# Second feed-forward on one core: VectorE takes the third pair's first sums between two softmaxes, and GpSimd waits for a tile's norm ahead of the next low part

## The chip, the cores and the metric

One core of a Trainium2 chip runs the whole program. The metric is the device time of one execution in microseconds (us), the median of the runs; less is better. A difference of under 0.2% (1.8 us here) counts as no change.

## The reference, cut to what matters

Attention with a decaying state gives 3072 tokens of 512 numbers. The first feed-forward follows (512 to 2048, ELU, back to 512), and then the second one, which the change is about:

```python
h = x @ w_in                                   # 3072 x 512 @ 512 x 1024
e = np.exp(h - np.max(h, axis=-1, keepdims=True))
solu = h * e / (np.sum(e, axis=-1, keepdims=True) + 1e-09)
mu = np.mean(solu, axis=-1, keepdims=True)
var = np.mean((solu - mu) ** 2, axis=-1, keepdims=True)
ln = (solu - mu) / np.sqrt(var + 1e-06) * g_ln
return ln @ w_out                              # 1024 x 512
```

## The kernel before, in words

Every matmul of the feed-forwards is split: an operand is a high part (rounded to the matmul's format by a ScalarE copy) plus a low part (the rest, a subtraction on VectorE or GpSimd), and each product is three matmuls: high with high, high with low, low with high.

The second feed-forward goes over 12 pairs of tiles of 128 tokens, `u` or `p` for a pair and `t` for a tile. Its first matmul is done by a scheme with seven products in place of eight for the four quarters of `h` (Strassen's, in Winograd's form). Products and sums of a pair `u` are these:

- TensorE, `up_product` (L513 to L521), six matmuls each: `opening_products` (P1 into bank X, P6 into bank Y), `middle_products` (P2 into X, P5 into W, then P7 into Y, which waits for the sum U2), `last_products` (P4 into Y, which waits for the sum U3, then P3 into W, which waits for H22).
- ScalarE copies P1 out (`copy_p1`, L925) and the first quarter of `h` (`copy_h2`, L932).
- VectorE, `add` (L710 to L712): `first_sums` makes U2 from P1 and bank Y, U3 from P1 and Y after P7, and H22 from U3 and bank W. `last_sums` makes H21 and H12.

Then each tile goes through `solu_max` (L816, L818), the exponential on ScalarE (L980), `solu_product` (L823), `solu_moments` (L829 to L838), the reciprocal root on GpSimd (`rstd`, L393) and `solu_normalise` (L845, L847, L849). TensorE transposes it (`norm_transposes`, L593, banks 4 and 5), ScalarE copies the high part (L990), VectorE takes the low part (`normalised_lo`, L805), and `solu_down` (L607 to L609, two halves of 12 matmuls) multiplies by the second weights.

Each engine runs its own list in the order written. TensorE's for a pair `p`, which makes the products of pair `p+1` between the transposes of tiles `2p` and `2p+1`, is: opening products, middle products, transposes of `2p`, last products, transposes of `2p+1`, four halves of `solu_down`. At `p = 0` the first tile's `solu_down` comes ahead of the transposes of tile 1, and the opening products of pair 2 follow those; at `p = 1` the list so begins with the middle products of pair 2. `norm_transposes(t)` waits for the tile's norm (semaphore `soft`, 13 counts for each tile) and for both low parts of the tile before (`nl_done`), since they are read from the same banks. VectorE's list has all of `first_sums(p+1)` at the start of pair `p`, behind both softmaxes of the pair before.

GpSimd makes the four sums of the input of a pair (`sum_x2`, L375, L378, L380, L383) and its low part (`split_x2_lo`, L388), both from SBUF, between the `rstd` of tiles. The low part also frees `x2_raw`, on which SyncE's load of the next input waits (`load_x2`, L299). Its sums come next in GpSimd's list, ahead of the next pair's two `rstd`.

Of the kernel before, what the change touches and what calls it, by code (L numbers as in the profile page):

```python
# [21 lines left out]
NT = TOK // P  # L22
NPAIR = NT // 2
# [10 lines left out]
def build(nc, units, w1, w_in2, w_out2, g_ln, tables, x2_dram, out):  # L34
# [4 lines left out]
    with ctx:  # L39
# [190 lines left out]
        SOFT = 13  # L230
# [9 lines left out]
        def sums(u, i):  # L240
            return 5 * u + i
# [105 lines left out]
        @block.gpsimd  # L347
        def _(pool):
            nc.gpsimd.memset(warm[:, :], 0.0).then_inc(warm_zeroed, 1)
            nc.gpsimd.memset(minus_half[:, :], -0.5).then_inc(consts_set, 1)  # L350

            def decay_q(n):
                pool.wait_ge(qk_in[slot(n)], 16 * loads(n))
                qt = tile_of(n)[:, QT]
                nc.gpsimd.tensor_tensor(qt, qt, q_decay[:, :], ALU.mult).then_inc(q_decayed, 1)  # L355

            def decay_v(n):
                pool.wait_ge(kv_in[slot(n)], 16 * loads(n))
                v = tile_of(n)[:, VN].rearrange("p (h d) -> p h d", d=D)
                nc.gpsimd.tensor_tensor(v, v, v_decay[:, :].unsqueeze(2).to_broadcast([P, H, D]), ALU.mult)\  # L360
                    .then_inc(v_decayed, 1)

            pool.wait_ge(q_decay_in, 16)
            decay_q(0)
            pool.wait_ge(v_decay_in, 16)
            decay_v(0)
            for n in range(1, NCH):
                decay_q(n)
                decay_v(n)

            def sum_x2(u):

                z = 4 * u
                pool.wait_ge(x2_in, 16 * (u + 1))
                nc.gpsimd.tensor_tensor(x2_raw[:, S3, :], x2_raw[:, A11, :], x2_raw[:, S1, :], ALU.subtract)\  # L375
                    .then_inc(x2_summed, 1)
                pool.wait_ge(x2_summed, z + 1)
                nc.gpsimd.tensor_tensor(x2_raw[:, S1, :], x2_raw[:, S1, :], x2_raw[:, A22, :], ALU.add).then_inc(x2_summed, 1)  # L378
                pool.wait_ge(x2_summed, z + 2)
                nc.gpsimd.tensor_tensor(x2_raw[:, S2, :], x2_raw[:, S1, :], x2_raw[:, A11, :], ALU.subtract)\  # L380
                    .then_inc(x2_summed, 1)
                pool.wait_ge(x2_summed, z + 3)
                nc.gpsimd.tensor_tensor(x2_raw[:, S4, :], x2_raw[:, A12, :], x2_raw[:, S2, :], ALU.subtract)\  # L383
                    .then_inc(x2_summed, 1)

            def split_x2_lo(u):
                pool.wait_ge(x2h_done, u + 1)
                nc.gpsimd.tensor_tensor(x2_lo[u % 2], x2_raw, x2_hi[u % 2].bitcast(f32), ALU.subtract).then_inc(x2l_done, 1)  # L388

            def rstd(t):  # L390
                par = t % 2
                pool.wait_ge(soft[par], SOFT * (t // 2) + 10)
                nc.gpsimd.tensor_tensor(stats[par][:, 8:9], stats[par][:, 7:8], minus_half[:, :], ALU.pow)\  # L393
                    .then_inc(rstd_done[par], 1)

            def scale_w4(k):
                pool.wait_ge(w4_in[k], 16)
                part = w_raw[:, W4 + 2 * k:W4 + 2 * k + 2, :]
                nc.gpsimd.tensor_tensor(part, part, gln_sb[:, 2 * k:2 * k + 2].unsqueeze(2).to_broadcast([P, 2, 512]),
                                        ALU.mult).then_inc(w4_scaled, 1)  # L400

            pool.wait_ge(consts_set, 1)
            pool.wait_ge(gln_in, 32)
            sum_x2(0)
            split_x2_lo(0)
            sum_x2(1)
            split_x2_lo(1)
            for k in range(4):
                scale_w4(k)
            sum_x2(2)  # L410
            split_x2_lo(2)
            rstd(0)
            rstd(1)
            for p in range(NPAIR - 1):
                if 0 < p < NPAIR - 2:
                    split_x2_lo(p + 2)
                if p + 3 < NPAIR:
                    sum_x2(p + 3)
                rstd(2 * p + 2)
                rstd(2 * p + 3)  # L420
# [225 lines left out]
        def _(dve):  # L646
# [63 lines left out]
            def add(out_, u, i, kept, bank, needs):  # L710
                dve.wait_ge(product, products(u, needs))
                nc.vector.tensor_tensor(out_, kept, bank, ALU.add).then_inc(h2_summed, 1)  # L712
# [83 lines left out]
            def last_sums(u):  # L796

                add(h2[:, 1, 0:512], u, H21, p1[:, :], Y, P4)
                add(h2[:, 0, 512:1024], u, H12, u2[:, :], W, P3)

            def normalised_lo(t):
                for q in range(2):
                    dve.wait_ge(nh_done, 2 * t + q + 1)
                    part = slice(q * (NF2 // 2), (q + 1) * (NF2 // 2))
                    nc.vector.tensor_tensor(n_lo[:, t % 2, part, :], ps[:, 4 + q, :].rearrange("p (f t) -> p f t", t=P),  # L805
                                            n_hi[:, t % 2, part, :].bitcast(f32), ALU.subtract).then_inc(nl_done, 1)
# [4 lines left out]
            def solu_max(t):  # L811
                u, done = t // 2, soft[t % 2]
                if t % 2 == 0:
                    dve.wait_ge(h2_copied, u + 1)
                dve.wait_ge(h2_summed, sums(u, H12))
                nc.vector.reduce_max(column(t, 0), h2[:, t % 2, :], AX.X).then_inc(done, 1)  # L816
                dve.wait_ge(done, SOFT * u + 1)
                nc.vector.tensor_scalar(column(t, 1), column(t, 0), -1.0, None, ALU.mult).then_inc(done, 1)  # L818

            def solu_product(t):  # L820
                par = t % 2
                dve.wait_ge(exp_done[par], t // 2 + 1)
                nc.vector.tensor_tensor(e3[:, par, :], e3[:, par, :], h2[:, par, :], ALU.mult).then_inc(soft[par], 1)  # L823

            def solu_moments(t):
                u, par, done = t // 2, t % 2, soft[t % 2]
                z = SOFT * u
                esum, esum_eps, r, r2, v = (column(t, n) for n in (2, 3, 4, 5, 7))
                nc.vector.tensor_scalar(esum_eps, esum, EPS_SM, None, ALU.add).then_inc(done, 1)  # L829
                dve.wait_ge(done, z + 4)  # L830
                nc.vector.reciprocal(r, esum_eps).then_inc(done, 1)
                for q in range(2):
                    nc.vector.bn_stats(bn[par][:, 6 * q:6 * q + 6], e3[:, par, 512 * q:512 * q + 512]).then_inc(done, 1)
                dve.wait_ge(done, z + 7)
                nc.vector.tensor_tensor(r2, r, r, ALU.mult).then_inc(done, 1)
                nc.vector.bn_aggr(mv[par][:, :], bn[par][:, :]).then_inc(done, 1)
                dve.wait_ge(done, z + 9)
                nc.vector.tensor_scalar(v, mv[par][:, 1:2], r2, EPS_LN, ALU.mult, ALU.add).then_inc(done, 1)  # L838

            def solu_normalise(t):  # L840
                u, par, done = t // 2, t % 2, soft[t % 2]
                z = SOFT * u
                r, rs, a, nb = (column(t, n) for n in (4, 8, 9, 10))
                dve.wait_ge(rstd_done[par], u + 1)
                nc.vector.tensor_tensor(a, rs, r, ALU.mult).then_inc(done, 1)  # L845
                dve.wait_ge(done, z + 11)
                nc.vector.tensor_scalar(nb, mv[par][:, 0:1], a, -1.0, ALU.mult, ALU.mult).then_inc(done, 1)  # L847
                dve.wait_ge(done, z + 12)
                nc.vector.tensor_scalar(e3[:, par, :], e3[:, par, :], a, nb, ALU.mult, ALU.add).then_inc(done, 1)  # L849
# [18 lines left out]
            add(h2[:, 1, 0:512], 1, H21, p1[:, :], Y, P4)  # L868
            solu_normalise(1)
            add(h2[:, 0, 512:1024], 1, H12, u2[:, :], W, P3)  # L870
            for p in range(NPAIR):
                t = 2 * p
                if 0 < p:
                    if p < NPAIR - 1:
                        first_sums(p + 1)
                        normalised_lo(t)
                        last_sums(p + 1)
                normalised_lo(t + 1)
                if p < NPAIR - 1:
                    solu_max(t + 2)  # L880
                    solu_max(t + 3)
                    for n in (t + 2, t + 3):
                        solu_product(n)
                        solu_moments(n)
                        if n == NT - 1:
                            normalised_lo(NT - 2)
                        solu_normalise(n)

        @block.scalar
        def _(act):  # L890
# [217 lines left out]
```

## Time and profile before

| what | value |
|---|---|
| median of 3 runs | 900.86 us (900.52 to 901.19) |
| the profiled execution | 900.97 us, of which the span is 899.2 us |
| TensorE matmul busy | 882.3 us (98%) |
| VectorE busy | 454.7 us (51%) |
| ScalarE busy | 327.7 us (36%) |
| GpSimd busy | 171.2 us (19%) |
| granted TensorE clock, mean over the span | 0.994 |

1.77 us of the profiled execution lie outside the span. Busy shares are means over the whole span; the change touches the stretch from about 630 us on.

### The profile page before, as it was taken

The numbers are of one execution on the slowest core, as the hardware profiler recorded it, in microseconds if no ns is written. First come the engines' busy times: TensorE is split into PE (matmuls) and PEld (weight loads), VectorE is DVE, ScalarE is ACT, GpSimd is POOL, SyncE is SP. The second block draws the span as 40 slices with busy tenths as digits, with TensorE's granted clock in tenths as the row PEclk, the third lists the DMA queues.
The fourth block names the chain that finished last, engine by engine and source line by source line (L and its number), as shares of the span: only waits on it lengthen the run. The fifth ranks groups of instructions, "written<-read, shape, count | busy, mean of one in ns | idle before, by whom it ended". The sixth has DMA issues, their size and how long they took to land.

```text
span 899.2 us, 12162 instructions
## 1 busy us (share of the span) xinstructions
PE 882.3 (98%) x4998; PEld 719.1 (80%) x4998; DVE 454.7 (51%) x755; ACT 327.7 (36%) x524; POOL 171.2 (19%) x142
## 2 busy tenths in 40 slices
PE   8999999999999999999999999999969999999998
PEld 5788888888888888888888888888858888888886
DVE  4765533332423332233423333485877777777774
ACT  2545332322423233332323244653323333333332
POOL 4221101110101111110200025211133333333200
PEclk9999999999999999999999999999979999999999
DMA  9900131110400131110400022401101111111001
GB/s 345 408 30 33 47 94 47 47 49 1 141 23 26 47 94 47 47 47 1 141 1 1 1 71 71 163 1 36 51 32 47 48 47 48 47 48 47 24 24 47
DMA packets 34006, 57.80 MB, mean 64 GB/s; under 512 B 2848, under 2 KB 15392, under 8 KB 33952
## 3 DMA queue, kind: packets, MB, share of 16 engines
q1 hardware_dynamic: 33376, 56.70, 18.2%
q8 instruction: 39, 0.64, 0.3%
q10 hardware_dynamic: 576, 0.33, 0.1%
q14 instruction: 15, 0.12, 0.0%
HBM read 44.44 MB, written 12.58 MB: 63 GB/s over the span
## 4 chain that ended last, share of the span: by engine, by line
PE 94%; DVE 4%; POOL 1%; issue 1%; DMA 0%; ACT 0%; POOLq 0%; ACTq 0%
PE ps L506 11%; PE ps L510 10%; PE ps L507 10%; PE ps L484 10%; PE ps L485 9%; PE ps L490 9%; PE ps L607 4%; PE ps L609 4%; PE ps L608 4%; PE ps L518 4%; PE ps L520 4%; PE ps L519 4%; PE ps L438 3%; PE ps L469 3%; PE ps L593 2%; PE ps L466 1%
## 5 line engine op out<-in xcount | busy, mean ns | idle before, releaser
L732 DVE TENSOR_TENSOR g_lo<-e,g_hi 128x512 fp32r<-128x512 f32 x96 | 76.7, 799 | 168.5 <-ACT g_hi L951 168.2
L506 PE MATMUL ps<-g_hi,w_hi 128*128 128x512 f32 x384 | 154.1, 401 | 0.0
L484 PE MATMUL ps<-x_hi,w_hi 128*128 128x512 f32 x384 | 149.9, 390 | 0.9 <-ACT x_hi L908 0.7
L510 PE MATMUL ps<-g_lo,w_hi 128*128 128x512 f32 x384 | 150.0, 391 | 0.0
L507 PE MATMUL ps<-g_hi,w_lo 128*128 128x512 f32 x384 | 149.7, 390 | 0.0
L485 PE MATMUL ps<-x_hi,w_lo 128*128 128x512 f32 x384 | 149.5, 389 | 0.0
L951 ACT ACTIVATE g_hi<-e 128x512 fp32r<-128x512 f32 x96 | 60.7, 632 | 202.7 <-PE ps L510 184.6
L725 DVE SCALAR_TENSOR_TENSOR e<-e,ps 128x512 f32<-128x512 f32 x96 | 65.7, 684 | 132.0 <-ACT e L942 132.0
L940 ACT ACTIVATE e<-ps 128x512 f32<-128x512 f32 x96 | 57.3, 597 | 141.9 <-PE ps L490 141.1
L355 POOL TENSOR_TENSOR tiles<-tiles,q_decay 128x512 f32<-128x512 f32 x23 | 31.8, 1383 | 384.1 <-DMA tiles<-units_dram 378.1
L490 PE MATMUL ps<-x_lo,w_hi 128*128 128x512 f32 x384 | 102.6, 389 | 0.0
L506 PEld LDWEIGHTS ps<-g_hi,w_hi 128*128 128x128 f32 x384 | 72.1, 188 | 17.9 <-issue 0.7
L484 PEld LDWEIGHTS ps<-x_hi,w_hi 128*128 128x128 f32 x384 | 72.1, 188 | 16.8 <-ACT x_hi L908 0.9
L510 PEld LDWEIGHTS ps<-g_lo,w_hi 128*128 128x128 f32 x384 | 72.1, 188 | 15.4
L490 PEld LDWEIGHTS ps<-x_lo,w_hi 128*128 128x128 f32 x384 | 72.1, 188 | 14.9
L485 PEld LDWEIGHTS ps<-x_hi,w_lo 128*128 128x128 f32 x384 | 72.1, 188 | 14.8
L507 PEld LDWEIGHTS ps<-g_hi,w_lo 128*128 128x128 f32 x384 | 72.2, 188 | 14.0
L607 PE MATMUL ps<-w_hi,n_hi 128*128 128x512 f32 x192 | 76.1, 396 | 0.0
L518 PE MATMUL ps<-w_hi,x_hi 128*128 128x512 f32 x168 | 67.7, 403 | 8.3 <-DVE u L712 8.3
L609 PE MATMUL ps<-w_hi,n_lo 128*128 128x512 f32 x192 | 75.0, 390 | 0.0
L608 PE MATMUL ps<-w_lo,n_hi 128*128 128x512 f32 x192 | 74.7, 389 | 0.0
L520 PE MATMUL ps<-w_hi,x_lo 128*128 128x512 f32 x168 | 66.1, 393 | 0.0
(84 smaller groups left out, 1165.2 us busy)
## 6 DMA issues: line engine op xcount, KB each, us to landing
tiles<-units_dram SPq DMA_DIRECT2D x46, 512.0 KB, 4.8
w_raw<-w_dram SPq DMA_DIRECT2D x32, 256.0 KB, 10.0
x_between<-x SPq DMA_DIRECT2D x24, 256.0 KB, 2.7
x_raw<-x_between SPq DMA_DIRECT2D x12, 512.0 KB, 3.5
out_dram<-y_sb SPq DMA_DIRECT2D x24, 256.0 KB, 2.0
w_raw<-w_out_dram SPq DMA_DIRECT2D x4, 512.0 KB, 3.7
w_raw<-w_in_dram SPq DMA_DIRECT2D x4, 512.0 KB, 5.3
tile<-units_dram SPq DMA_DIRECT2D x2, 512.0 KB, 10.9
```

Source lines behind the costliest of these rows:

```text
L484: nc.tensor.matmul(bank, hi, x_hi[:, j % 2, k, :], start=(k == 0), stop=False)
L485: nc.tensor.matmul(bank, lo, x_hi[:, j % 2, k, :], start=False, stop=False)
L490: last = nc.tensor.matmul(bank, hi, x_lo[:, j % 2, k, :], start=False, stop=(k == KD - 1))
L506: nc.tensor.matmul(ps[:, 4 + m, :], hi, g_hi[:, f % 2, :], start=(f == 0), stop=False)
L507: nc.tensor.matmul(ps[:, 4 + m, :], lo, g_hi[:, f % 2, :], start=False, stop=False)
L510: last = nc.tensor.matmul(ps[:, 4 + m, :], hi, g_lo[:, f % 2, :], start=False, stop=(f == NF1 - 1))
L518: nc.tensor.matmul(bank, x_h, hi, start=(first and k == 0), stop=False, skip_group_check=True)
L520: done = nc.tensor.matmul(bank, x_l, hi, start=False, stop=(k == 1), skip_group_check=True)
L607: nc.tensor.matmul(bank, n_hi[:, par, f, :], hi, start=(f == 0), stop=False)
L608: nc.tensor.matmul(bank, n_hi[:, par, f, :], lo, start=False, stop=False)
L609: last = nc.tensor.matmul(bank, n_lo[:, par, f, :], hi, start=False, stop=(f == NF2 - 1))
L732: nc.vector.tensor_tensor(g_lo[:, f % 2, :], e[:, f % 2, :], g_hi[:, f % 2, :].bitcast(f32), ALU.subtract)\
```

## The change

VectorE takes U2 of pair 2 right after the norm of tile 2, and U3 and H22 of pair 2 between the moments and the norm of tile 3; before, all three stood behind the norm of tile 3. From pair 1 on, the maximum of the first tile of the next pair comes ahead of the low part of tile `2p+1`. GpSimd gets a wait for the norm of tile `2p+1` ahead of `split_x2_lo(p+2)`, for `p` from 1 to 9. The last low part is written behind the loop instead of in it. The instructions themselves, their number and their shapes stay as they are.

```diff
             for p in range(NPAIR - 1):
                 if 0 < p < NPAIR - 2:
+                    pool.wait_ge(soft[1], SOFT * (p + 1))
                     split_x2_lo(p + 2)
...
-            for p in range(NPAIR):
+            for p in range(NPAIR - 1):
                 t = 2 * p
-                if 0 < p:
-                    if p < NPAIR - 1:
+                if p > 0:
+                    if p > 1:
                         first_sums(p + 1)
-                        normalised_lo(t)
-                        last_sums(p + 1)
-                normalised_lo(t + 1)
-                if p < NPAIR - 1:
+                    normalised_lo(t)
+                    last_sums(p + 1)
+                if p > 0:
                     solu_max(t + 2)
-                    solu_max(t + 3)
-                    for n in (t + 2, t + 3):
-                        solu_product(n)
-                        solu_moments(n)
-                        if n == NT - 1:
-                            normalised_lo(NT - 2)
-                        solu_normalise(n)
+                    normalised_lo(t + 1)
+                else:
+                    normalised_lo(t + 1)
+                    solu_max(t + 2)
+                solu_max(t + 3)
+                solu_product(t + 2)
+                solu_moments(t + 2)
+                solu_normalise(t + 2)
+                if p == 0:
+                    dve.wait_ge(p1_copied, 3)
+                    add(u2[:, :], 2, U2, p1[:, :], Y, P6)
+                solu_product(t + 3)
+                solu_moments(t + 3)
+                if p == 0:
+                    add(u3[:, :], 2, U3, p1[:, :], Y, P7)
+                    dve.wait_ge(h2_summed, sums(2, U3))
+                    add(h2[:, 1, 512:1024], 2, H22, u3[:, :], W, P5)
+                if p == NPAIR - 2:
+                    normalised_lo(NT - 2)
+                solu_normalise(t + 3)
+            normalised_lo(NT - 1)
```

## Rows read from the trace of the kernel before

**Rows 1.** The page: granted TensorE clock in 40 slices, tenths.
```profile
PEclk9999999999999999999999999999979999999999
```
**Rows 2.** The waits of TensorE from 590 us on: total, times, longest.
```profile
PE ps L518 <- DVE u L712: 8.3, 2, 7.9
```
**Rows 3.** The timeline of TensorE: start, length, instruction, idle time before it.
```profile
650.02 0.39 PE L518 MATMUL ps<-w_hi,x_hi 128*128 128x512 f32 x1
...
652.51 0.39 PE L520 MATMUL ps<-w_hi,x_lo 128*128 128x512 f32 x1
...
660.77 0.79 PE L518 MATMUL ps<-w_hi,x_hi 128*128 128x512 f32 x1 [7.87 <-DVE u L712]
...
880.12 1.09 PE L593 MATMUL ps<-ident,e 128*128 128x128 f32 x8 [1.14 <-DVE e L849]
```
**Rows 4.** Busy time by stretch; then granted clock, DMA share, GB/s.
```profile
660.70:665.00 4.30, 4.23 (x14) 3.55 (x15) 1.25 (x3) 0.42 (x1) 2.19 (x3) 0.50 0.24 90
...
690.54:712.95 22.41, 22.41 (x109) 18.59 (x107) 16.82 (x35) 8.53 (x13) 8.10 (x7) 1.00 0.13 47
...
876.00:888.00 12.00, 10.86 (x56) 8.61 (x55) 8.56 (x24) 3.97 (x8) 1.09 (x2) 1.00 0.11 44
```
**Rows 5.** The timeline of VectorE at the norms of tiles 2 and 3.
```profile
650.50 0.81 DVE L849 TENSOR_SCALAR e<-e,stats 128x1024 f32<-128x1024 f32 x1
651.23 1.22 DVE L823 TENSOR_TENSOR e<-e,h 128x1024 f32<-128x1024 f32 x1
...
654.24 0.21 DVE L838 TENSOR_SCALAR stats<-mv,stats 128x1 f32<-128x1 f32 x1
655.12 3.90 DVE L845 TENSOR_TENSOR stats<-stats 128x1 f32<-128x1 f32 x1 [0.67 <-POOL stats L393]
...
660.03 0.68 DVE L712 TENSOR_TENSOR u<-p,ps 128x512 f32<-128x512 f32 x1
```
**Rows 6.** The instructions of L845: minimum, median and maximum in ns.
```profile
L845 DVE TENSOR_TENSOR stats<-stats x24: 149/159/3902, 629.6 to 884.3; 128x1 f32<-128x1 f32 x24
```
**Rows 7.** The timeline of GpSimd in the same stretch.
```profile
649.47 0.55 POOL L393 TENSOR_TENSOR stats<-stats,minus_half 128x1 f32<-128x1 f32 x1 [8.87 <-DVE stats L838]
...
655.05 3.95 POOL L388 TENSOR_TENSOR x_lo<-x_raw,x_hi 128x1792 fp32r<-128x1792 f32 x1
662.66 0.74 POOL L375 TENSOR_TENSOR x_raw<-x_raw 128x256 f32<-128x256 f32 x1 [3.65 <-DMA x_raw<-x_between]
...
665.08 0.73 POOL L383 TENSOR_TENSOR x_raw<-x_raw 128x256 f32<-128x256 f32 x1
```
**Rows 8.** The chain that ended last, in order of time.
```profile
632.63 0.50 PE ps L518
...
663.69 1.68 PE ps L593 x8
...
668.13 0.87 PE ps L593 x8
```
**Rows 9.** The timeline of VectorE: two low parts back to back.
```profile
633.21 1.28 DVE L805 TENSOR_TENSOR n_lo<-ps,n_hi 128x512 fp32r<-128x512 f32 x2
```
**Rows 10.** The groups of VectorE over the whole span: count, busy and mean.
```profile
L816 DVE TENSOR_REDUCE stats<-h 128x1 f32<-128x1024 f32 x24 | 29.0, 1209 | 0.1
```
**Rows 11.** The timeline of VectorE and GpSimd one pair later, undisturbed.
```profile
682.54 0.82 DVE L849 TENSOR_SCALAR e<-e,stats 128x1024 f32<-128x1024 f32 x1
...
686.77 0.69 DVE L712 TENSOR_TENSOR u<-p,ps 128x512 f32<-128x512 f32 x1 [2.81 <-PE ps L520]
...
683.59 4.03 POOL L388 TENSOR_TENSOR x_lo<-x_raw,x_hi 128x1792 fp32r<-128x1792 f32 x1 [1.53 <-ACT x_hi L973]
```
**Rows 12.** VectorE beside GpSimd's input sums, in the first feed-forward's end.
```profile
583.39 1.77 DVE L740 TENSOR_TENSOR w_lo<-w_raw,w_hi 128x1024 fp32r<-128x1024 f32 x1
...
584.15 1.61 POOL L380 TENSOR_TENSOR x_raw<-x_raw 128x256 f32<-128x256 f32 x1
```
**Rows 13.** The timeline of VectorE at the last pair, ahead of the softmaxes.
```profile
871.01 1.29 DVE L805 TENSOR_TENSOR n_lo<-ps,n_hi 128x512 fp32r<-128x512 f32 x2 [0.38 <-ACT n_hi L990]
```

## The prediction

> **What bounds the kernel now.** I read the page first, for where TensorE is not at its limit. It is busy for 98% of the span, and its granted clock is full but in one slice of 40, the 30th, a little after 652 us [rows 1]. The waits of TensorE from 590 us on say why: it stood still twice for VectorE's first sums, 8.3 us in all, of which one time is 7.9 us [rows 2]. The timeline has that wait at 652.9 to 660.77 us, ahead of the first matmul of P7 of pair 2 [rows 3]. In the stretch behind it the clock is 0.50, its lower level of 1.2 GHz; in an undisturbed pair it is 1.00 and TensorE is busy for all of 22.41 us [rows 4]. So the kernel is bound by TensorE, and there is one hole in it.
>
> What made the hole is in VectorE's rows. U2 of pair 2 ran only at 660.03, behind the whole softmax of tile 3 [rows 5]. Its inputs were old by then: bank Y was complete before the middle products began at 650.02. VectorE spent 3.90 us of that time in L845, a product of two 128x1 columns, whose median over 24 is 0.159 us [rows 5, 6]. GpSimd's low part ran from 655.05 to 659.00, and L845 ended at 659.02 [rows 5, 7]. So a VectorE operation with two inputs from SBUF stands still until the GpSimd operation that began before it is over.
>
> **Part 1: U2 ahead of the product of tile 3.** The norm of tile 2 starts at 650.50 and the next operation 0.73 later, 0.08 before its end [rows 5]. By that, U2 (0.68 us) runs from 651.23 to 651.91. TensorE gets to P7 after the 12 matmuls of P2 and P5: 650.02 + 12 x 0.2265 = 652.74, where 0.2265 is (652.51 - 650.02) / 11 [rows 3]. U2 is 0.8 us early, so the wait of 7.87 us goes. P7 takes 6 x 0.2265 = 1.36 us to 654.10, and the eight transposes of tile 2, whose norm and banks are long ready, 0.87 us to 654.97; at the low clock these took 1.68 [rows 8].
>
> **What is late next: U3.** The last products of pair 2 wait for U3, which now stands behind the product and the moments of tile 3. All these slide by U2's 0.60: the moments end at 654.45 + 0.60 = 655.05 [rows 5], and U3 runs from 654.97 to 655.66. With 0.06 from U2's end (660.71) to the start of P7 (660.77) [rows 3, 5], P4 starts at 655.72, so TensorE is idle for 0.75 us. A first matmul after such a hole takes 0.50 in the chain in place of 0.23 [rows 8]. P4 and P3: 655.72 + 12 x 0.2265 + 0.27 = 658.71. H22 ends at 656.4, in time for P3.
>
> **What is late after that: the low part of tile 2.** The transposes of tile 3 need its norm and both low parts of tile 2. After H22 the norm starts with L845 at 656.4. By the wait of part 2 no long GpSimd operation stands in front of it. From the root's end (649.47 + 0.55) to the start of L849 there are 0.48 us [rows 5, 7], and L849 takes 0.81: 657.7. The two low parts take 1.28 more, 0.08 overlapped [rows 9]: 658.90, and TensorE gets going at 658.95, a second hole of 0.24 us.
>
> **The sum.** The transposes of tile 3 began at 668.13 [rows 8] and would begin at 658.95, 9.2 us earlier. Checked from the other side: 8.03 for the wait (652.74 to 660.77) and 2.37 for the low clock and the restart (from 660.77 to the end of the transposes at 665.37 are 4.60, where 1.36 + 0.87 are due), less 0.75 and 0.24 of new holes and 0.27 for their restart, is 9.1. From there TensorE's list is the same work, so all of it reaches the end if no later wait takes it back.
>
> **Part 2: GpSimd's wait.** In pair 1 it puts the low part of pair 3 from 655.05 to 657.75, and its 4.0 us then lie beside VectorE's low parts of tile 2, H21, H12 and a maximum. None of these has two SBUF inputs; an add of the same kind took its usual 0.69 beside a GpSimd low part of 4.03 [rows 11], so I cost the overlap at nothing. Queued behind the waiting low part are the load of pair 4's input on SyncE, its four sums, and the two roots of tiles 4 and 5. From the old rows, the load takes 662.66 - 659.00 = 3.66 us and the sums 665.81 - 662.66 = 3.15 [rows 7]: low part 657.75 to 661.8, sums 665.4 to 668.6. The root of tile 4 is asked for at 667.3: the low parts of tile 2, H21 and H12 end at about 660.2, a maximum is 1.21 [rows 10], and with both maxima, the low parts of tile 3 and the product and moments (3.22 from 651.23 to 654.45) [rows 5] I get 667.3. It comes 1.2 us later. U2 of pair 3 follows at 668.6 + 1.8 (root to norm) + 3.1 + 1.9 + 0.65 = 676.05. TensorE comes to P7 of pair 3 at 658.95 + 0.87 + 48 x 0.2265 + 24 x 0.2265 = 676.1. That is a tie; I take 0.1 us as lost, and 0 to 1.5 as its bounds. Product and sums also meet on SBUF: in the one place where they did before, VectorE's took 1.77 and a sum 1.61 [rows 12], against 1.22 for a product of that size alone [rows 5] and 0.73 for a sum [rows 7]. Only a column product of the moments falls among the sums here, and the root waits for their end anyway.
>
> In the following pairs the wait costs nothing: in the undisturbed pair the norm of the odd tile was over at 683.36 and the low part began at 683.59, held by ScalarE's copy [rows 11]. By the load and the sums above, the sums end at 683.59 + 4.03 + 3.66 + 3.15 = 694.4. The next root is due 22.41 after that of tile 4, which ran 1.03 + 5.1 ahead of 682.54 (root to L849 as in [rows 5, 7], and from norm to norm), so at 698.8, 4.4 us later.
>
> **Part 3: the maximum ahead of the low part of tile 2p+1.** It fills the 0.38 us in which VectorE waited for ScalarE's copy [rows 13], and brings the softmax forward by up to that. The low part comes 0.9 us later; its reader, `solu_down` of the odd tile, comes 24 matmuls (5.4 us) behind the transposes, so this is free. In the pairs where TensorE has no wait the gain is 0. At the end it has one of 1.14 us, for the norm of tile 22 [rows 3]: gain 0 to 0.38, I take 0.25.
>
> **Together:** 900.97 - 9.2 + 0.1 - 0.25 = 891.6 for an execution like the profiled one, whose own time is 0.1 above the median of the runs: 891.5 us.
>
> **A rule that speaks against it.** Two short holes replace a long one. In this trace a hole of 1.14 us left the granted clock at 1.00 [rows 3, 4]. The Trainium skill ("TensorE: Matmul & The Clock Gate", section "A second HAM failure mode: psum-queue depth-cycling") says that frequent short idle times between groups of matmuls can make the clock swing between its levels. By the row nothing is lost; by the rule the time would be that of the first rival.
>
> **The rivals.**
> - *The clock falls in the new holes.* They are 3.0 us apart and together 1.0 us, less than the one that did no harm. Price: the slow stretch measured here, 2.1 us (4.60 against 2.5). 893.6 us. Chance 7%.
> - *The wait moves to pair 3.* The tie above falls the wrong way, because the load lands later or the sums and VectorE's product hold each other up. Each us of lateness is a us of TensorE. With 1 to 2 us: 893.0. Nothing in the rows is that late, but the slack is nil. Chance 10%.
> - *The low part blocks VectorE in its new place too.* If the low parts of tile 2 (one input in PSUM, one in SBUF) stood still beside it, they would end at 661.8 + 1.3 = 663.1 and the gain would be 9.2 - 4.2 = 5.0: 895.7 us. Against it is the add of [rows 11], of the same kinds of operands. Chance 4%. The Trainium skill ("SBUF — State Buffer", section "Who interferes with whom") leaves this rival nothing, since it lets an operation with one SBUF input go beside GpSimd; the trace agrees where it shows such a pair.
> - *Nothing is gained*, since P7 has another late input: 900.9. All its other inputs are in use by the products before it. Chance 1%.
> - *Slower:* the wait delays GpSimd's queue in each pair. The root has 4.4 us to spare there, and U2 1.4 more (it ends at 682.54 + 0.73 + 0.68 = 683.95, and P7 comes at 668.13 + 0.87 + 72 x 0.2265 = 685.3). If the way from the low part's start to the sums' end were not 10.8 us but 18.0, then 1.4 us would be lost in each of nine pairs, 12.6 in all: 904.1 us. From 17.9 on the kernel is slower by over 0.2%. Chance 1%.
>
> **How the numbers follow.** The forecast has 77%. Its own bounds: both new holes closed and the whole 0.38 give 890.5, the tie at its bad end 893.0. The range takes in the first two rivals: 890.6 to 893.6; outside it stay the last three rivals, 6%, and the far ends of the others. Faster by over 0.2% (about what a measurement of this kernel can tell from no change) is every case but the last two, less something for what I have not seen: 0.96; same 0.02; slower 0.02.
>
> **What would show it.** TensorE: P7 of pair 2 starts at 652.7 with no wait, and new waits stand before the last products (0.75, for U3) and the transposes of tile 3 (0.24, for the low part). VectorE: no L845 over 0.7 us. GpSimd: the first low part of the loop starts at 657.7, the root of tile 4 directly behind the last sum. TensorE's wait for tile 22 is 0.9. The full clock in each slice from the 28th on. The prediction is wrong if a wait of over 1 us stands before P7 of pair 3, or the clock falls at 655.

## The result and the profile after

The changed kernel takes 891.33 us in the median of 4 runs (890.54 to 892.95), against 900.77 for the kernel before beside it: a ratio of 0.9897, 95% interval 0.988 to 0.9914, so about 1.0% faster. The forecast was 891.5. The profiled execution took 891.14 us, its span is 889.3 us. Of all the runs reported here one, of e9_u3_behind_norm, took 1094.26 us at a mean granted clock of 0.753; it is left out of that kernel's median and ratio.

The page's slices of the changed kernel, TensorE's busy tenths and its granted clock:

```profile
PE   8999999999999999999999999999999999999998
...
PEclk9999999999999999999999999999999999999999
```

The slice of [rows 1] that had a low clock is gone. TensorE's waits from 590 us on, after (line numbers in the changed kernel are 2 higher from TensorE's part on: L520 is L518 of before, L595 is L593, L714 is L712, L807 is L805, L847 is L845, L851 is L849):

```profile
PE ps L520 <- DVE u L714: 1.0, 2, 0.6
PE ps L595 <- DVE e L851: 0.8, 1, 0.8
PE ps L595 <- DVE n_lo L807: 0.2, 1, 0.2
```

Against [rows 2] the two waits for VectorE's sums went from 8.3 to 1.0 us, and a new one of 0.2 us for a low part has come. TensorE's timeline shows where: P7 of pair 2 starts at 652.44 straight behind the matmul before it, P4 waits for U3, the transposes of tile 3 for the low part of tile 2, and those of tile 22 for the norm, where [rows 3] had 1.14 us.

```profile
652.44 0.39 PE L520 MATMUL ps<-w_hi,x_hi 128*128 128x512 f32 x1
...
655.39 0.50 PE L520 MATMUL ps<-w_hi,x_hi 128*128 128x512 f32 x1 [0.55 <-DVE u L714]
...
658.57 1.06 PE L595 MATMUL ps<-ident,e 128*128 128x128 f32 x8 [0.16 <-DVE n_lo L807]
...
870.32 1.09 PE L595 MATMUL ps<-ident,e 128*128 128x128 f32 x8 [0.81 <-DVE e L851]
```

VectorE's timeline of the same stretch, to be held against [rows 5]. U2 stands behind the norm of tile 2; the column product L847 takes 0.15 us where it took 3.90. The low parts of tile 2 take their usual 1.28 us.

```profile
650.19 0.81 DVE L851 TENSOR_SCALAR e<-e,stats 128x1024 f32<-128x1024 f32 x1
650.92 0.68 DVE L714 TENSOR_TENSOR u<-p,ps 128x512 f32<-128x512 f32 x1
651.52 1.22 DVE L825 TENSOR_TENSOR e<-e,h 128x1024 f32<-128x1024 f32 x1
...
654.66 0.68 DVE L714 TENSOR_TENSOR u<-p,ps 128x512 f32<-128x512 f32 x1
655.37 0.69 DVE L714 TENSOR_TENSOR h<-u,ps 128x512 f32<-128x512 f32 x1
655.98 0.15 DVE L847 TENSOR_TENSOR stats<-stats 128x1 f32<-128x1 f32 x1
...
656.41 0.81 DVE L851 TENSOR_SCALAR e<-e,stats 128x1024 f32<-128x1024 f32 x1
657.14 1.28 DVE L807 TENSOR_TENSOR n_lo<-ps,n_hi 128x512 fp32r<-128x512 f32 x2
```

GpSimd's timeline, against [rows 7]. The low part of pair 3 starts right after the norm, at 657.31, and the sums behind it in the list, those of the next input, end at 668.19, with the root of tile 4 directly after them. The last row is the low part of pair 4: in [rows 11] it was ScalarE's copy that released it, here it is the norm of tile 5.

```profile
657.31 4.06 POOL L388 TENSOR_TENSOR x_lo<-x_raw,x_hi 128x1792 fp32r<-128x1792 f32 x1 [1.93 <-DVE e L851]
665.01 0.74 POOL L375 TENSOR_TENSOR x_raw<-x_raw 128x256 f32<-128x256 f32 x1 [3.64 <-DMA x_raw<-x_between]
...
667.46 0.73 POOL L383 TENSOR_TENSOR x_raw<-x_raw 128x256 f32<-128x256 f32 x1
668.15 0.55 POOL L393 TENSOR_TENSOR stats<-stats,minus_half 128x1 f32<-128x1 f32 x1
...
675.14 4.03 POOL L388 TENSOR_TENSOR x_lo<-x_raw,x_hi 128x1792 fp32r<-128x1792 f32 x1 [1.37 <-DVE e L851]
```

This execution is 0.31 us ahead of the one before already at the norm of tile 2 (650.19 against 650.50), from work that the change does not touch. The transposes of tile 3 are over at 658.57 + 1.06 = 659.63; before, they were over at 668.13 + 0.87 = 669.00 [rows 8]. That is 9.37 us earlier, of which 9.06 come on top of the 0.31. With the last wait shorter by 0.33 these make 9.70 of the 9.9 us of the span. Of the other 0.2, about 0.1 gathers in the pairs between, where TensorE has no wait in either trace; its cause is open.

### The profile page after: what moved, and what is told of

It is laid out like the page before. It is cut to its first block, busy times and chain, and to the rows that moved or that the text cites. A ratio compares the mean times of both kernels' runs of the same rounds, so it can differ in the third digit from the quotient of the medians.

```text
span 889.3 us, 12171 instructions
## 1 busy us (share of the span) xinstructions
PE 880.0 (99%) x4998; PEld 717.1 (81%) x4998; DVE 450.3 (51%) x755; ACT 327.6 (37%) x524; POOL 170.5 (19%) x142
## 4 chain that ended last, share of the span: by engine, by line
PE 94%; DVE 4%; issue 1%; POOL 1%; DMA 0%; ACT 0%; POOLq 0%; DVEq 0%; ACTq 0%
PE ps L508 11%; PE ps L512 10%; PE ps L509 10%; PE ps L486 10%; PE ps L487 10%; PE ps L492 10%; PE ps L609 4%; PE ps L610 4%; PE ps L611 4%; PE ps L520 4%; PE ps L522 4%; PE ps L521 4%; PE ps L440 3%; PE ps L471 3%; PE ps L595 2%; PE ps L468 1%
## 5 line engine op out<-in xcount | busy, mean ns | idle before, releaser
L520 PE MATMUL ps<-w_hi,x_hi 128*128 128x512 f32 x168 | 67.0, 399 | 1.0 <-DVE u L714 1.0
```

Of the source, the lines that this page charges most:

```text
L520: nc.tensor.matmul(bank, x_h, hi, start=(first and k == 0), stop=False, skip_group_check=True)
```

## The experiments

Nine kernels, each compared with the kernel before on the same chip; medians.

| kernel | what differs | us |
|---|---|---|
| e1_sums_only | changed kernel, no GpSimd wait, no swap of maximum and low part | 895.15 |
| e2_wait_only | kernel before, GpSimd's wait alone | 896.95 |
| e3_no_swap | changed kernel, no swap | 891.50 |
| e4_swap_only | kernel before, the swap alone | 900.38 |
| e5_one_wait | changed kernel, GpSimd's wait in pair 1 alone | 896.29 |
| e6_u2_in_gap | changed kernel, U2 one place further ahead | 890.67 |
| e7_gap_and_pair1 | e6, and U3 of pair 1 ahead of a product | 890.75 |
| e8_two_waits | changed kernel, GpSimd's wait in pairs 1 and 2 | 891.19 |
| e9_u3_behind_norm | changed kernel, U3 and H22 back behind the norm | 893.14 |

**e1_sums_only.** Does the new place of the sums do the work alone?

```diff
-                    pool.wait_ge(soft[1], SOFT * (p + 1))
...
-                if p > 0:
-                    solu_max(t + 2)
-                    normalised_lo(t + 1)
-                else:
-                    normalised_lo(t + 1)
-                    solu_max(t + 2)
+                normalised_lo(t + 1)
+                solu_max(t + 2)
```

> The changed kernel without GpSimd's wait and without the maximum ahead of the low part: only U2, U3 and H22 of pair 2 stand at their new places. Theory (VectorE stands still beside a GpSimd operation that reads SBUF): GpSimd's low part starts at about 655.3, right behind the root of tile 3; U3 and H22 run, the column product of the norm of tile 3 is held until about 659.4, the transposes of tile 3 start near 661.8 instead of 658.6. 3.2 us lost there and 0.3 at the end: 894.9 us; 2 us more if the clock falls in the 3.5 us hole. Rival (the 3.9 us of that column product was a wait for something else, which U2's old place brought about): 891.6 us, and no column product over 0.7 us.

Measured: 895.15 us, ratio 0.9941 (0.9926 to 0.9955). The column product is held until GpSimd's low part is over, and TensorE waits 3.43 us ahead of the transposes of tile 3. VectorE's, GpSimd's and TensorE's timelines of this kernel:

```profile
656.35 3.42 DVE L846 TENSOR_TENSOR stats<-stats 128x1 f32<-128x1 f32 x1
```

```profile
655.72 4.03 POOL L388 TENSOR_TENSOR x_lo<-x_raw,x_hi 128x1792 fp32r<-128x1792 f32 x1
```

```profile
662.21 1.06 PE L594 MATMUL ps<-ident,e 128*128 128x128 f32 x8 [3.43 <-DVE n_lo L806]
```

Both ended within 0.02 us of each other (659.77 and 659.75). The rival, by which the long column product came from U2's old place, falls. In this hole the clock stayed up (1.00 in the windows from 658 to 664 us), so the lower of the theory's two figures was due, and it came. Against e3_no_swap below, which differs from e1 by GpSimd's wait alone, the wait is worth 3.65 us here.

**e2_wait_only.** The other half alone.

```diff
                 if 0 < p < NPAIR - 2:
+                    pool.wait_ge(soft[1], SOFT * (p + 1))
                     split_x2_lo(p + 2)
```

> The kernel before with GpSimd's wait alone. Theory: the column product of tile 3 takes 0.16 us, U2 of pair 2 runs at about 656.3 instead of 660.03, TensorE's wait for it shrinks from 7.9 to about 4.1 us. 895.0 us if the clock stays up in the shorter hole, 897.1 if it falls as before. Rival (the hole comes from U2's place alone, the wait on GpSimd only avoids damage that the new place would do): 900.8 us.

Measured: 896.95 us, ratio 0.9962 (0.9948 to 0.9976). The hole is 4.12 us and the clock fell in it, as the second stretch shows (start and end; length; busy by engine; granted clock, DMA share, GB/s):

```profile
652.60:656.70 4.10, 0.08 (x1) 0.00 (x0) 3.29 (x9) 0.07 (x1) 1.02 (x2) 0.95 0.00 0
656.70:660.70 4.00, 3.90 (x15) 3.13 (x16) 0.94 (x3) 0.44 (x1) 3.53 (x1) 0.62 0.00 0
```

That is the theory's figure for a fallen clock, 897.1, and the rival's 900.8 falls. GpSimd's wait is worth 3.8 us by itself, without any move of the sums. The gains of e1 (5.6) and of e2 (3.8) add up to nearly the whole, but each alone leaves another hole: of 3.43 us behind P3 in e1, of 4.12 us ahead of P7 and with a clock price in e2.

**e3_no_swap and e4_swap_only.** The maximum ahead of the low part of tile 2p+1, taken out of the changed kernel and put alone into the kernel before. e3's edit is the second hunk of e1's; e4's is this:

```diff
-                normalised_lo(t + 1)
-                if p < NPAIR - 1:
+                if 0 < p < NPAIR - 1:
+                    solu_max(t + 2)
+                normalised_lo(t + 1)
+                if p == 0:
                     solu_max(t + 2)
+                if p < NPAIR - 1:
                     solu_max(t + 3)
```

> The changed kernel with the low part of tile 2p+1 ahead of the maximum again. Theory: TensorE's wait for the norm of tile 22 is 1.1 us again instead of 0.8, all else stays: 891.6 us, 0.3 more than the changed kernel. Rival (the earlier maximum also helps pair 3, where GpSimd's sums are late): a wait of TensorE before P7 of pair 3, 892 us or more.

> The kernel before with the maximum of the next even tile ahead of the low part of tile 2p+1, from pair 1 on, and nothing else. Theory: the 7.9 us hole stays, only TensorE's last wait (1.14 us) shrinks by 0.3: 900.5 us, which can't be told from no change by the time, only in the trace. Rival (the swap carries part of the gain): under 899 us.

Measured: 891.50 (0.9899, 0.9884 to 0.9914) and 900.38 us (0.9996, 0.9986 to 1.0005). Neither can be told by the time from the kernel it is to be held against. The traces tell them: TensorE's wait for the norm of tile 22, first in e3 and then, below its long wait for U2, in e4,

```profile
PE ps L595 <- DVE e L851: 1.2, 1, 1.2
```

```profile
PE ps L518 <- DVE u L712: 8.3, 2, 7.9
PE ps L593 <- DVE e L849: 0.8, 1, 0.8
```

so the swap is worth 0.3 to 0.4 us at the last pair and nothing in front of it. In e3 no wait stands before P7 of pair 3, so e3's rival falls.

**e5_one_wait.** Are the waits of the pairs behind the first needed?

```diff
                 if 0 < p < NPAIR - 2:
-                    pool.wait_ge(soft[1], SOFT * (p + 1))
+                    if p == 1:
+                        pool.wait_ge(soft[1], SOFT * (p + 1))
                     split_x2_lo(p + 2)
```

> The changed kernel with GpSimd's wait in pair 1 alone; the other eight waits are left out. Theory (in later pairs the low part is held by ScalarE's copy, which ends after the norm, or nearly so): the same time as the changed kernel, 891.3 us. Rival (the norm of pair 2's odd tile is now so late that its low part would start ahead of it and hold it): 892 us or more, with a long column product at about 673.8.

Measured: 896.29 us, ratio 0.9944 (0.9924 to 0.9964), 5.0 more than the changed kernel. The theory fell here and the rival held. GpSimd's, VectorE's and TensorE's timelines:

```profile
674.25 3.99 POOL L388 TENSOR_TENSOR x_lo<-x_raw,x_hi 128x1792 fp32r<-128x1792 f32 x1 [0.49 <-ACT x_hi L990]
```

```profile
673.98 0.21 DVE L850 TENSOR_SCALAR stats<-mv,stats 128x1 f32<-128x1 f32 x1
674.23 4.55 DVE L852 TENSOR_SCALAR e<-e,stats 128x1024 f32<-128x1024 f32 x1
678.71 0.68 DVE L715 TENSOR_TENSOR u<-p,ps 128x512 f32<-128x512 f32 x1
```

```profile
679.44 0.80 PE L521 MATMUL ps<-w_hi,x_hi 128*128 128x512 f32 x1 [3.42 <-DVE u L715]
```

ScalarE's copy released the low part at 674.25, while the norm of tile 5, 1.2 us late behind GpSimd's sums, was at its very start. What was held is not the column product, as the rival had it, but the long TENSOR_SCALAR that follows it in the norm, recorded from 674.23 and over only at 678.78, where 0.81 is usual. The norm's recorded start is 0.02 us ahead of GpSimd's, and it was held all the same; so these starts don't tell which of two such operations will be held. U2 of pair 3 was late, and P7 of pair 3 with it: the tie that the prediction found, tipped by 3.4 us. The rest of the 5.0 us goes with the clock, which was at 0.51 behind this hole (last section): from the start of P7 of pair 3 to that of P4 are 3.86 us here (679.44 to 683.30) and 2.33 in the changed kernel (675.84 to 678.17).

**e8_two_waits.** The same with the wait in pairs 1 and 2 (`if p <= 2:`).

> The changed kernel with GpSimd's wait in pairs 1 and 2 only; the seven others are left out. Theory (in pair 2 the wait counts because the norm of its odd tile comes late, behind GpSimd's sums; from pair 3 on ScalarE's copy is the later one): 891.3 us, no norm over 1.1 us. Rival (each wait counts a little): between 891.8 and 896.

Measured: 891.19 us, ratio 0.9891 (0.9875 to 0.9908), and no norm over 1.07 us: the instructions of its line, minimum, median and maximum in ns:

```profile
L852 DVE TENSOR_SCALAR e<-e,stats x24: 811/812/1068, 629.8 to 875.0; 128x1024 f32<-128x1024 f32 x24
```

Of the nine waits, two carry the gain, and the seven others nothing that can be measured.

**e9_u3_behind_norm.** Is it U3 that comes late next?

```diff
-                if p == 0:
-                    add(u3[:, :], 2, U3, p1[:, :], Y, P7)
-                    dve.wait_ge(h2_summed, sums(2, U3))
-                    add(h2[:, 1, 512:1024], 2, H22, u3[:, :], W, P5)
                 if p == NPAIR - 2:
                     normalised_lo(NT - 2)
                 solu_normalise(t + 3)
+                if p == 0:
+                    add(u3[:, :], 2, U3, p1[:, :], Y, P7)
+                    dve.wait_ge(h2_summed, sums(2, U3))
+                    add(h2[:, 1, 512:1024], 2, H22, u3[:, :], W, P5)
```

> The changed kernel with U3 and H22 of pair 2 behind the norm of tile 3 again; only U2 keeps its new place, and GpSimd its wait. Theory (after U2 it is U3 that sets the last products): U3 ends at about 657.3 instead of 655.3, TensorE waits 2.5 us there instead of 0.55, the low part of tile 2 no longer binds, and the transposes of tile 3 come 1.75 us later: 893.1 us. Rival (the low part of tile 2, at the end of the same list, sets the end anyway): 892.1 us, by the 0.75 us that it comes later.

Measured: 893.14 us, ratio 0.9914 (0.9898 to 0.9931), 1.8 more than the changed kernel; the theory gave 1.8 and the rival 0.8. TensorE's timeline has the wait of the theory:

```profile
657.63 0.50 PE L520 MATMUL ps<-w_hi,x_hi 128*128 128x512 f32 x1 [2.49 <-DVE u L714]
```

**e6_u2_in_gap and e7_gap_and_pair1.** Can the holes that are left be closed? In e6 U2 of pair 2 goes ahead of the norm of tile 2, into the wait for GpSimd's root, as U2 of pair 1 already does. e7 adds an edit in pair 1.

```diff
-                solu_normalise(t + 2)
                 if p == 0:
                     dve.wait_ge(p1_copied, 3)
                     add(u2[:, :], 2, U2, p1[:, :], Y, P6)
+                solu_normalise(t + 2)
```

```diff
-            solu_product(1)
             add(u3[:, :], 1, U3, p1[:, :], Y, P7)
+            solu_product(1)
+            dve.wait_ge(soft[1], 3)
             dve.wait_ge(h2_summed, sums(1, U3))
```

> The changed kernel with U2 of pair 2 one place further ahead: between the moments and the norm of tile 2, in the 0.66 us in which VectorE waits for GpSimd's root. Theory (both small holes left in TensorE, 0.55 and 0.2 us, follow from VectorE's list): U2 costs VectorE nothing there, all behind it comes 0.6 us earlier, and both holes shrink to 0.1 or less: 890.7 us. Rival (TensorE is held there by its own list, the products before P7): no gain, 891.3.

> As the one with U2 in the gap, and U3 of pair 1 ahead of the product of tile 1, with a wait for that product ahead of H22. Theory: U3 of pair 1 runs at about 631.3 instead of 631.6 to 632.3, TensorE's wait of 0.46 us before the last products of pair 1 goes, and up to 0.2 comes back before P3: another 0.3, 890.4 us. Rival (VectorE waits 0.3 us more for P7 and passes it on through the norm of tile 1): 890.7, no better than the one before.

Measured: 890.67 us (0.9881, 0.9863 to 0.9898) and 890.75 us (0.9882, 0.9864 to 0.99). e6's chain has the transposes of tile 3 at 658.10; from the end of the moments of tile 2 (649.20 there, 649.08 after) they are 8.90 us away and not 9.49, so the 0.6 us of the theory are in the trace, and of TensorE's waits only these are left:

```profile
PE ps L595 <- DVE e L851: 0.8, 1, 0.8
PE ps L520 <- DVE u L714: 0.5, 1, 0.5
```

The medians agree with it (0.66 us less than the changed kernel), but the intervals overlap, so that e6 is faster is shown by the trace and not by the clock of the runs. e7's trace has the wait of 0.46 us gone and waits of 0.2 ahead of P3 of pair 1 and of 0.2 for the low part of tile 2 in its place:

```profile
PE ps L520 <- DVE h L714: 0.2, 1, 0.2
PE ps L595 <- DVE n_lo L807: 0.2, 1, 0.2
```

Between pair 1's U2 and the transposes of tile 3 e7 is 0.1 us shorter than e6; the expected 0.3 did not come, and the time shows nothing of it.

## Why the prediction was right, and where it was not

**The hole and its two causes.** Right. The wait before P7 of pair 2 went whole. That its causes were two, U2's place and GpSimd's low part in front of the column product, is shown by e1 and e2, which each leave one standing.

**U3 is late next, then the low part of tile 2.** Right in place and order: predicted waits 0.75 and 0.24, measured 0.55 and 0.16. P4 itself started where it was forecast: at 655.39, against 655.72 less the 0.31 by which this execution is ahead. The wait shown is shorter than my 0.75, since it counts from the end of the last transpose's record (653.81 + 1.04), and I counted the transposes by the 0.87 us that they take in the chain. The transposes of tile 3 started 0.07 us earlier than forecast, since VectorE's norm started 0.61 us behind H22's start (655.37 to 655.98) and not 0.7. e9 confirms that U3 sets the last products. The sum was 9.2 us. By the starts of the transposes of tile 3 (668.13, 658.57) it is 9.25; by their ends, which are what TensorE's list goes on from, 9.06. The sum left out that a stretch behind a wait restarts: these transposes took 1.06 us and not 0.87.

**The cost of the overlap beside the low part of pair 3: nothing.** Right; the low parts of tile 2 ran 1.28 us beside it, as in [rows 9]. But the test behind it, whether an operation has two inputs in SBUF, was too narrow. e5's norm has one input tensor there and was held. No such norm fell beside a low part in the changed kernel. The rival that they would be held falls. "SBUF — State Buffer", "Who interferes with whom", in the Trainium skill says that an operation with at most one SBUF input, outside the two-port modes, does not contend; this row agrees. It also names `tensor_scalar` as one that can enter a two-port mode and then does contend. e5's norm of 4.55 us fits that, but no view of the trace shows the mode.

**The tie before P7 of pair 3.** Right, and nearer than it was comfortable: U2 ended at 675.66 and P7 started at 675.84 with no wait. I took 0.1 us as lost, and it was 0.

**"In the following pairs the wait costs nothing."** Right as to cost. But the paragraph looked at the pair as it was before, undisturbed, and took from it that the wait also does nothing there. In pair 2 the root that my own sum had 1.2 us late pushes the norm behind ScalarE's copy, and there the wait is worth 5.0 us (e5). The number of the forecast was not touched, since the wait is in the change also for pair 2. That is luck: the mechanism was missed, and with it 5.0 us of the gain hung on a wait that the paragraph took to do nothing. From pair 3 on the paragraph holds (e8).

**The swap.** Predicted 0.25 with bounds 0 to 0.38, measured 0.33 between the traces of before and after, and 0.36 between the waits of e3 (1.17) and after (0.81).

**The clock.** The rival did not come about in the profiled execution: its mean granted clock is 1.000. By the Trainium skill, "TensorE: Matmul & The Clock Gate", section "A second HAM failure mode: psum-queue depth-cycling", frequent short idle times between groups of matmuls made the clock swing in a kernel; two of 0.55 and 0.16 us did not do it here. Of the three other runs the longest, 892.95 us, has a mean of 0.998. It left no trace of its own, so whether its clock fell in the new holes is open. The same mean stands in the traces of e1 and e7 for another reason: there the clock is at 0.50 between 9 and 11 us, far ahead of the change.

**The slower rival.** Nothing of it: no pair behind the second has a wait of TensorE at all, until the last.

**The bounds.** With both holes closed, the whole 0.38 and nothing lost at the tie, the prediction's own terms give 891.5 - 0.99 - 0.13 - 0.1 = 890.3, and not the 890.5 that it states. The measured median is not near that end.

## What to carry to other kernels

When an engine's short operation takes as long as what is left of a long GpSimd operation beside it, it is being held, and what is to be asked is not only where the waiting work stands but what GpSimd is allowed to start in front of it; here a wait on GpSimd, with nothing else, gave 0.4%. Having moved a long operation back, follow its queue one round further: its own successors came 1.2 us late and made a second meeting, which the same wait happened to prevent. A list's idle time while it waits for a small result of another engine (0.66 us for a root) is the place for a sum that something else is waiting for.

## What the runs showed of the hardware

A GpSimd operation of 4.03 us that reads two tiles in SBUF held a VectorE product of two 128x1 columns, which took 3.42 us in place of 0.16 (e1). One of 3.99 us held a TENSOR_SCALAR of 128x1024 with one input tensor in SBUF, which took 4.55 us in place of 0.81 (e5). Not held beside such an operation were an add and a subtraction with one input in PSUM (0.69 us in e1, 1.28 us for two in the changed kernel) and a maximum over 128x1024 (1.22 us).

Short operations hold each other as well, and either side can be the one that pays. At the norm of tile 1, in both kernels, VectorE's column product takes 0.68 to 0.69 us and the TENSOR_SCALAR 1.07 beside the sums of GpSimd, and one of these sums takes 1.07 us where 0.74 is usual.

Holes of nearly one length ended in different clocks. After 3.43 us in e1 the transposes ran at full clock; after 3.42 us in e5 the clock was 0.51, its lower level, for the next stretch. The windows of e1 and then of e5:

```profile
662.20:664.20 2.00, 1.99 (x13) 1.82 (x14) 1.75 (x4) 1.09 (x2) 0.75 (x1) 1.00 0.12 46
```

```profile
679.40:682.00 2.60, 2.56 (x6) 2.07 (x7) 0.00 (x0) 0.00 (x0) 0.02 (x1) 0.51 0.63 202
```

Of a hole of that length one can't say ahead whether it costs 1 to 2 us more. Behind the holes of 2.49 us and less in the traces the clock was at its full level. That is no proof of a safe length: in the kernel before it is 0.99 in the window from 654 to 655 us and 0.50 in the next, so it fell 2.1 us after TensorE had come to a stop at 652.9. What decides when it falls was not tried.
